# Recurrence and gated layer written as one program, with the attention's first batch kept on the chip

## The reference

```python
for t in range(S):                                   # recurrence
    cur = einsum('bhd,bhe->bhde', u[None] * kt, vt)
    y[:, :, t] = einsum('bhd,bhde->bhe', rt, state + cur)
    state = wt[:, :, :, None] * state + einsum('bhd,bhe->bhde', kt, vt)
...
h = maximum(x @ w_in, 0)                             # gated layer, w_in 384 x 1024
conv_out = sum over k of conv_w[k] * shifted(h, k)   # 3 taps over tokens
z = h * sigmoid(conv_out) @ w_out                    # w_out 1024 x 384
...
q, k, v = z @ wq[e], z @ wk[e], z @ wv[e]            # 4 experts, 64 wide each
a = softmax(causal(scale * q @ k.T))
out += top2_weight[e] * (a @ v @ wo[e])
```

## Time and profile before

| | us |
|---|---|
| median of 3 runs | 671.43 |
| lowest, highest | 671.18, 677.67 |
| the profiled execution | 671.61 |
| its span, first to last instruction | 669.9 |

### The profile page before, as it was taken

One profiled execution on the slowest core, in us unless ns is written; L12 is line 12 of the kernel. 1 busy time (PEld: TensorE's weight loads), 2 busy tenths in 40 slices (PEclk: granted clock), 3 DMA queues, 4 the chain that ended last, 5 costly groups with the idle time before them and its releaser, 6 DMA issues. The chain is left out here.

```text
span 669.9 us, 11883 instructions
## 1 busy us (share of the span) xinstructions
PE 598.4 (89%) x4505; PEld 492.7 (74%) x4505; DVE 425.5 (64%) x747; ACT 352.2 (53%) x812; POOL 130.3 (19%) x142
## 2 busy tenths in 40 slices
PE   1899989992799999999999649799999999999886
PEld 0777767772799999999999549576677767676545
DVE  6799999944556666666666342655764665456653
ACT  2557656755556656655665332544643454343540
POOL 1444444401000000000000010422232133132330
PEclk9989989996899999999999859899999999999999
DMA  8459899417200030040010050200000210001001
GB/s 346 147 104 207 173 327 199 134 38 190 82 0 1 37 105 1 1 141 0 0 71 1 0 212 1 70 1 1 27 23 13 83 37 13 13 13 48 13 12 71
DMA packets 22263, 49.55 MB, mean 74 GB/s; under 512 B 6924, under 2 KB 14500, under 8 KB 21348
## 3 DMA queue, kind: packets, MB, share of 16 engines
q1 hardware_dynamic: 22212, 48.85, 24.8%
HBM read 34.69 MB, written 14.16 MB: 73 GB/s over the span
## 5 line engine op out<-in xcount | busy, mean ns | idle before, releaser
L1042 POOL TENSOR_SCALAR att_a<-att_a,att_rden,att_gate 128x128 f32<-128x128 f32 (+5 forms) x96 | 68.4, 722 | 191.8 <-DVE att_rden L1181 191.8
L1173 DVE TENSOR_REDUCE att_nmax<-att_ps 128x1 f32<-128x128 f32 (+5 forms) x96 | 55.2, 617 | 52.3 <-PE att_ps L1290 52.3
L73 PE MATMUL hid_ps<-hid_g_lo,hid_w_hi 128*128 128x384 f32 x192 | 67.2, 350 | 6.3 <-DVE hid_g_lo L803 6.2
L73 PE MATMUL hid_ps<-hid_x_lo,hid_w_hi 128*128 128x384 f32 x192 | 66.4, 346 | 6.2 <-ACT hid_conv_sb L766 5.4
L793 DVE SCALAR_TENSOR_TENSOR hid_cv<-hid_h,hid_conv_sb,hid_cv 128x768 f32<-128x768 f32 x64 | 65.0, 1016 | 2.4 <-ACT hid_cv L726 1.2
L75 PE MATMUL hid_ps<-hid_g_hi,hid_w_hi 128*128 128x384 f32 x192 | 66.0, 344 | 0.0
L74 PE MATMUL hid_ps<-hid_g_hi,hid_w_lo 128*128 128x384 f32 x192 | 66.0, 344 | 0.0
L74 PE MATMUL hid_ps<-hid_x_hi,hid_w_lo 128*128 128x384 f32 x192 | 65.8, 343 | 0.0
L75 PE MATMUL hid_ps<-hid_x_hi,hid_w_hi 128*128 128x384 f32 x192 | 65.7, 342 | 0.0
L1071 ACT ACTIVATE att_a<-att_ps,att_nmax 128x128 f32<-128x128 f32 (+5 forms) x96 | 59.9, 633 | 3.9 <-DVE att_nmax L1173 3.6
L1081 ACT ACTIVATE att_at<-att_ps 128x512 f32<-128x512 f32 (+2 forms) x64 | 27.1, 449 | 63.9 <-PE att_ps L1315 63.6
(11 more groups left out here) (145 smaller groups left out, 1326.6 us busy)
## 6 DMA issues: line engine op xcount, KB each, us to landing
rec_kr<-in_kr_img SPq DMA_DIRECT2D x10, 576.0 KB, 10.0
rec_kr<-in_kr_img SPq DMA_DIRECT2D x3, 1536.0 KB, 9.2
rec_v_n<-in_v_img SPq DMA_DIRECT2D x8, 576.0 KB, 10.9
x_features<-rec_x_p SPq DMA_DIRECT2D x16, 288.0 KB, 10.4
hid_x_t<-x_features SPq DMA_DIRECT2D x12, 384.0 KB, 5.3
z_features<-hid_z_t SPq DMA_DIRECT2D x4, 1152.0 KB, 4.8
att_z_t<-z_features SPq DMA_DIRECT2D x12, 384.0 KB, 4.3
out_y<-att_o_sb SPq DMA_DIRECT2D x24, 192.0 KB, 1.9
```

What stands on the lines that cost most here:

```text
L73: nc.tensor.matmul(dst, xh, yl, start=start, stop=False, skip_group_check=True)
L1042: G.tensor_scalar(probs, probs, rden[:, t:t + 1], gate[:, b % 2, 2 * ep + odd, i:i + 1], ALU.mult, ALU.mult).then_inc(a_scaled, 1)
L1173: V.tensor_reduce(nmax[:, t:t + 1], ps[:, lo:lo + n], AX_X, ALU.max, negate=True).then_inc(nmax_ready, 1)
```

## The change

- `recurrence` and `hidden` become one program, `features`. What the second needs before it can start is placed among the last chunks: ScalarE makes the high parts of the weights in six pieces behind chunks 12 to 17, VectorE the low parts of w_in behind chunks 19 and 20 and those of w_out behind chunk 23, x of batch 0 is loaded behind `store(5)` and split by ScalarE behind chunks 20 and 21 and by VectorE behind chunks 21 and 22, and TensorE makes `make_h(0, 0)` ahead of `output(23)`. GpSimd makes no low parts; it zeroes the two border columns of h.
- The rows of the convolution are loaded at the start and turned between `gather(0)` and `scores(1)`, into bank 3; ScalarE copies them out ahead of `own(1)`, and `scores(1)` waits for that.
- The loop over batches is written out. Tiles share room: the kr slots hold x and later the attention's weights, the raw weights hold h, z and one cv.
- The attention's weights are loaded behind the last x store. z of batch 0 is loaded back, during batch 2 of the layer, into the room of `x_p` (`spare`).
- The attention starts with batch 0 of z there; its order is z, then wv and wo, then wq and wk. The first four projections (q and k of the first pair) take the unsplit tiles and one full float32 multiply instead of three of rounded halves. `c_ready` is waited for behind the projections.

```diff
 # features (was recurrence and hidden): SP
+            weights.load_conv(sp)
...
+                if hb == NB - 2:
+                    load_x(0)
             store(NB - 1)
+            load_next(sp)
+            for b in range(B):
+                if b + 1 < B:
+                    load_x(b + 1)
+                store_z(b)
+                if b == B - 2:
+                    sp.wait_ge(z_stored, 16 * (b + 1))
+                    sp.dma_start(spare[:, 0:FT * S].rearrange("p (t s) -> p t s", t=FT),
+                                 z_dram[0].rearrange("(t p) s -> p t s", p=P)).then_inc(z_first, 16)
...
 # GpSimd
+            pool.wait_ge(w_split, FT)
+            G.memset(h[:, :, 0:1], 0.0).then_inc(h_zero, 1)
+            G.memset(h[:, :, S + 1:S + 2], 0.0).then_inc(h_zero, 1)
...
 # ScalarE
             take_ks(0)
+            act.wait_ge(conv_psum, 1)
+            A.activation(conv_sb[:], bank[3][:, 0:3 * NF], ACT.Copy).then_inc(conv_ready, 1)
             own(1)
...
+                if N - C - NW <= i < N - C:
+                    split_w(i - (N - C - NW))
+                if N - 4 <= i < N - 2:
+                    split_x(0, i - (N - 4))
+            rectify(0, 0)
+            act.wait_ge(w_split, NW)
+            rectify(0, 1)
+            sigmoid(0, 0)
...
 # VectorE
+                if i == N - 5:
+                    split_w(0)
+                if i == N - 4:
+                    split_w(1)
+                    split_w(2)
+                if N - 3 <= i < N - 1:
+                    split_x(0, i - (N - 3))
+            for n in range(FT, NW):
+                split_w(n)
+            dve.wait_ge(conv_ready, 1)
+            convolve(0, 0)
...
 # TensorE
             gather(0)
+            turn_conv()
...
+                if i == N - 1:
+                    make_h(0, 0)
                 output(i)
...
 # attention: SP
-            load(0)
...
 # attention: ScalarE
-            A.activation(w_hi[:, 0:weights.WV], w_raw[:, 0:weights.WV], ACT.Copy).then_inc(w_split_hi, 1)
             for t in range(FT):
                 split_z(0, t)
             A.activation(w_hi[:, weights.WV:], w_raw[:, weights.WV:weights.N], ACT.Copy).then_inc(w_split_hi, 1)
+            A.activation(w_hi[:, 0:weights.WV], w_raw[:, 0:weights.WV], ACT.Copy).then_inc(w_split_hi, 1)
...
 # attention: TensorE, project_z
-                    if n == 0:
+                    if n == (4 if b == 0 else 0):
                         pe.wait_ge(z_lo_ready, FT * b + t + 1)
-                    if what == "v":
+                    if b == 0 and n < 4:
+                        m = mm(dst[:, 0:HALF], (whole_wq if what == "q" else whole_wk)[:, t, 0:P],
+                               first_z[:, t, HALF * where[1]:HALF * (where[1] + 1)], start=(t == 0), stop=(t == FT - 1),
+                               skip_group_check=True)
+                    elif what == "v":
...
-            pe.wait_ge(c_ready, 4)
+            pe.wait_ge(weights.loaded, weights.N_LOADED)
             for n in range(NPJ):
                 project_z(0, n)
+            pe.wait_ge(c_ready, 4)
```

More of the change, by code:

```diff
@@ L230, in load_kr @@
             def load_kr(hb):
-                s3 = hb % NKR
+                slot = hb % NKR
                 if hb >= NKR:
@@ L464, in mask, with prepare @@
+            def prepare(hb, stage):
+                if stage == 0:
+                    products(hb)
+                    scan(hb)
+                elif stage == 1:
+                    invert(hb)
+                    between_chunks(hb)
+                else:
+                    for part in range(3):
+                        decay(hb, part)
             def mask(i):
@@ L503, in _ @@
                     mask(i + 1)
[L504 to L510 removed]
+                if i < 2:
+                    prepare(1, i + 1)
+                if 2 <= hb < NB:
+                    prepare(hb, stage)
+                if i == N - 5:
[9 more added lines that the diff above has]
+            convolve(0, 0)
+            gate_hidden(0, 0)
+            for b in range(B):
+                last = b == B - 1
+                for f in range(NF):
+                    split_g(b, f)
+                    if f + 1 < NF or not last:
+                        convolve(b, f + 1)
+                    if f + LAG == NF - 1 and not last:
+                        split_x(b + 1, 0)
+                    if f + 1 < NF or not last:
+                        gate_hidden(b, f + 1)
+                    if f + LAG == NF - 1 and not last:
+                        split_x(b + 1, 1)
         @block.tensor
@@ new lines, in output, with turn_conv, make_h @@
+                m.then_inc(y_psum, 1)
+            def turn_conv():
+                pe.wait_ge(weights.s_conv, 16)
+                nc.tensor.transpose(bank[3][:, 0:3 * NF], weights.conv_rows[:, :], ident[0:3 * NF, 0:3 * NF]).then_inc(conv_psum, 1)
+            def make_h(b, f):
+                cols = slice(P * (f % NF), P * (f % NF + 1))
+                for half in range(2):
+                    tokens = slice(HALF * half, HALF * (half + 1))
+                    if b == 0 and f == 0:
+                        pe.wait_ge(w_split, FT)
+                        pe.wait_ge(ks_ready, step(N - 1))
+                        pe.wait_ge(bon_ready, NB)
+                        pe.wait_ge(st_ready, step(N - 1))
+                    wait(pe, h_ready, 2 * (NF * b + f) + half - 1)
+                    for t in range(FT):
+                        if f % NF == 0:
+                            pe.wait_ge(x_split, FT * (2 * (b + f // NF) + half) + t + 1)
+                        m = product(nc, bank[NZ + half][:, 0:HALF], (in_hi[:, t, cols], in_lo[:, t, cols]),
+                                    (x_hi[:, t, tokens], x_lo[:, t, tokens]), t == 0, t == FT - 1)
+                    m.then_inc(h_psum, 1)
@@ new lines, in add_z @@
+            def add_z(b, f):
+                if b == 0 and f == 0:
+                    pe.wait_ge(w_split, NW)
+                    pe.wait_ge(a_ready, 2 * N)
+                    pe.wait_ge(y_taken, N)
+                pe.wait_ge(g_split, NF * b + f + 1)
+                for n in range(NZ):
+                    cols, tokens = slice(P * (n // 2), P * (n // 2 + 1)), slice(HALF * (n % 2), HALF * (n % 2 + 1))
+                    if f == 0:
+                        wait(pe, z_taken, NZ * (b - 1) + n + 1)
+                    m = product(nc, bank[n][:, 0:HALF], (out_hi[:, f, cols], out_lo[:, f, cols]),
+                                (g_hi[:, f % 2, tokens], g_rest[:, f % 2, tokens]), f == 0, f == NF - 1)
+                m.then_inc(g_used, 1)
@@ L863, in batch, with attention @@
+            make_h(0, 1)
+            for b in range(B):
+                for f in range(NF):
+                    if f + LAG < NF or b + 1 < B:
                         make_h(b, f + LAG)
                     add_z(b, f)
-            pe.wait_ge(w_split, 1)
-            make_h(0, 0)
-            make_h(0, 1)
-            pe.wait_ge(w_split, 2)
-            each_batch_last(pe, B, batch)
-def attention(nc, z_dram, weights, out):
+def attention(nc, spare, z_dram, weights, out):
     B, F, S = z_dram.shape
@@ L937, in attention @@
         wo_parts = [weights.out_part(x) for x in (w_hi, w_lo)]
+        whole_wq, whole_wk = (weights.part(w_raw, start, E * HD) for start in (weights.WQ, weights.WK))
+        first_z = spare[:, 0:FT * S].rearrange("p (t s) -> p t s", t=FT)
         z_t = sb("z_t", [P, FT, S])
```

552 lines of the change are left out of this document (236 added, 316 removed).

## The result

| | before | after |
|---|---|---|
| median on one chip, us | 672.94 (4 runs) | 657.04 (4 runs) |
| lowest, highest | 671.18, 677.67 | 654.52, 658.51 |
| the profiled execution | 671.61 | 654.52 |
| its span | 669.9 | 652.8 |

The changed kernel takes 0.972 of the time before, with a 95% interval of 0.968 to 0.976. Some executions lie more than 1.5% above the fastest of their kernel; every ratio here leaves them out and is taken to the kernel before on the same chip. Forecast were 654.3 us and, for the profiled execution, a span of 652.8 us.

A forecast was written before the change was run, and what follows sets the result against it. VectorE bounds the recurrence, TensorE the gated layer; TensorE's stops between stages count. Span 669.9 - 13.3 - 3.8 = 652.8 us; plus 1.7 outside, less 0.2 to the median, 654.3 us; range 651 to 660.

The forecast's parts named there:

- The first seam: Recurrence to gated layer: TensorE's idling before the first add_z closes, 14.1 less 0.8 at the start, 13.3 us saved.
- The slack of 3.8 us: Behind the last chunk: VectorE's three w_out subtractions finish 3.8 us before rectify(0, 1) needs them, so they cost nothing.
- The start: Conv rows' transpose and copy before own(1) make the mask of chunk 1 0.8 us late, carried to the recurrence's end.
- The first seam's own 14.1: Saving at the recurrence-to-layer seam before the start's delay: add_z(0, 0) at 164.7 instead of 178.87, 14.1 us.
- The second seam: Gated layer to attention: TensorE starts 5.6 us earlier on unsplit tiles; 3.8 us saved, bounds -0.7 and 4.9.
- The size of the work: Attention's first four projections as 12 full fp32 multiplies of 384 columns: 8.0 us taken, 7.7 to 12.5 considered.
- The other price taken there: Whole scores, short columns included, priced at 1.16 ns a column; gave 10.7 us for the 12 fp32 multiplies.
- the lower clock: At the attention's start TensorE runs at 1.2 GHz for 5.3 us, adding half of it, 2.65 us.
- The second seam gives nothing: Rival at the attention's start: fp32 projections cost 12.5 us or split weights are late; 658 to 659 us, chance 0.12.
- The splits stretch the recurrence: Rival in chunks 12 to 17: ScalarE's six weight copies lie on the path, 5.5 us more, 660 us; chance 0.10.
- The written-out layer is slower: Rival in the gated layer: instruction-issue stalls decide from 16 on, 678 us with 22; chance 0.02.
- Half the first seam: Rival at the recurrence-to-layer seam: an unseen wait holds make_h(0, 0) or rectify(0, 1); 661 us or more, chance 0.04.

The follow-up runs named there:

- the four kernels: Attention's z from DRAM or kept on chip, first projections split or full float32; copies of z to first exp 36.85/36.81 and 36.68 split, 35.85 and 32.11 to 32.92 float32.

## Why the prediction held, step by step

- *The first seam, 13.3 us.* The add_z came at 165.62 and was forecast for about 165.5; 13.25 us were saved. Every intermediate time held to 0.8 us, most of it the late start: the first product at 148.97 ahead of output(23), the pause of 1.08 us (1.1), the subtractions from 149.74 to 153.2 (149.4 to 152.9), ScalarE's first copies at 154.98 (154.35), the second half of rectify(0, 1) at 159.00 (158.2). The pause did not lower the clock. The slack of 3.8 us was 4.2 at rectify(0, 1) and 3.7 at the convolution; of what the tripled subtractions took beyond it 2.2 us reached add_z and 0.65 the end of the layer.
- *The start, 0.8 us.* The mask was 0.63 us late, and 0.50 remained at the last mask, in two executions with the same mean clock. The mechanism at chunk 1 is shown by its removal (24.56). But the prediction carried the delay on unchanged, and it did not stay so: by VectorE's meeting with GpSimd it was 1.05 us from chunk 2 to chunk 15, and it fell to 0.5 because the kernel before met GpSimd at chunk 16. That the term of 0.8 came so near is luck. The first seam's own 14.1 was 13.75, and the two errors cancel.
- *The second seam, 3.8 us.* The mechanism was right and is shown by the four kernels: both halves are needed. The size of the work was 7.74 us for 8.0: the price taken from the long columns of the scores, 0.84 ns a column and record, was that of the new form to the last digit. The other price taken there was misread. The short part of those scores has 256 columns and not 128 (timeline of TensorE, kernel before):

```profile
435.10 0.60 PE L1286 MATMUL att_ps<-att_k_t,att_q_t 64*128 64x256 f32 x4
```

  With 1.49 us over two records of 512 and two of 256 columns it is 0.97 ns a column for the 1.16, and the upper end from it 8.9 us for the 10.7; the 8.0 that the sum took does not hang on it. The term that was mis-sized is the lower clock, 2.65 us: the first v product came 9.55 us behind the start, so it cost 1.8 us here, and 1.9 to 2.6 in the others with this attention (9.6 to 10.4 us). The first v product came 5.0 us earlier, counted from the copies of z, and the first exp 4.74 (14.95 us from the one to the other with the old order of the attention's start, 15.25 with the new one); the 0.65 us more behind it are within the scatter. The estimate of 8.4 us of work, made from what the Trainium skill says of true fp32 (FP8 and Floating Point Precision, TensorE Precision Notes), was 0.7 us too high, since it priced the four passes by the spacing of fp32r records; four passes agree with the row, as an estimate of 4 x 384 columns at 2.4 GHz, 0.64 us, stands beside 0.645 us measured.
- *The rivals.* "The second seam gives nothing": TensorE went on from the float32 products to v without a wait, VectorE was through at 383.4. "The splits stretch the recurrence": not in the change (its masks of chunks 12 to 17 come 1.05 to 0.5 us later, the delay of the start); the doubled copies cost 1.65 us of a possible 6.3. "The written-out layer is slower": add_z to the end of the layer 203.30 against 203.06 us, 0.2 us in these two executions. "Half the first seam": no wait was hidden there.
- *The time.* That the span came out to 0.1 us is partly luck: the profiled executions of both kernels had 0.96 in the recurrence, and the second seam saved 0.9 us more than forecast, which 0.24 us in the layer and 0.65 behind the first exp took back. The median of 657.04 us lies 2.7 us above the forecast. The other three executions have a lower mean clock (0.968 to 0.974 for 0.976); that this is the recurrence's, as in the profiled ones, is likely, but their stages are not on record.

## What to carry over

Follow one chain through a seam, from the last instruction that is not changed to the first that comes out the same, and price only what is new; the errors of such a sum were 0.3 to 1 us here. Where two waits end at nearly the same time, an edit that removes one is worth little by itself (0.2 and 1.0 of 4 us), so try the pair before dropping either. Before you give work to an idle engine, ask which busy one it can hold: GpSimd stopped a full VectorE for 6.5 us in order to save it 3.5. A small delay can grow where it shifts two engines against each other: 0.63 us became 1.08.

## What the runs showed that I had not expected

- GpSimd's subtraction holds back VectorE's products wholly: three times in a row, 0.55 us became 2.72 and twice 0.95 became 3.1.
- A full float32 multiply of 128 x 128 x 384 costs 0.645 us at full clock, against 3 x 0.176 = 0.53 for the three fp32r products it stands for. It is 22% dearer on TensorE and does not wait for the splits.
- A load of the function table lasts 1.28 us. Moved off ScalarE's path it gave 1.4 us back at the first seam and 1.0 at the second.
- TensorE's clock drops in the recurrence for a time that differs between executions, although TensorE is busy 9 of 10 us there; with a stall for issue in one of them, the last mask of the same program came between 147.1 and 152.4 us.
- A delay of 0.63 us at the start grew to 1.08 by the next mask, because two of VectorE's small products now met GpSimd's, where one had before.
